# One scan for all head pairs, the range test between the masks, and a new order behind chunk 11

## The reference

```python
for t in range(S):                                   # r, k, v, w: (2, 8, 768, 48)
    cur = einsum('bhd,bhe->bhde', u[None] * kt, vt)
    y[:, :, t] = einsum('bhd,bhde->bhe', rt, state + cur)
    state = wt[:, :, :, None] * state + einsum('bhd,bhe->bhde', kt, vt)
# x: y as (2, 768, 384)
h = gelu_tanh(x @ w_in); u, v = h[..., :512], h[..., 512:]
v_s = einsum('ts,bsd->btd', w_sg, normalise(v) * g_ln) + b_sg[None, :, None]
x = x + (u * v_s) @ w_out
u2 = x + (relu(x.T @ w_tok1) @ w_tok2).T
out = u2 + relu(u2 @ w_ch1) @ w_ch2
```

## Time and profile before

| | us |
|---|---|
| median of 3 runs | 390.93 |
| lowest, highest | 390.72, 392.92 |
| the profiled execution | 391.33 |
| its span (first to last instruction) | 389.8 |
| busy: PE, DVE, POOL, ACT | 379.3, 178.7, 178.2, 105.3 |

### The profile page before, as it was taken

How to read it: one execution, slowest core, us unless ns; L and a number is a source line. 1 busy time by engine, 2 the same in 40 slices (tenths; PEclk the granted TensorE clock), 3 DMA queues, 4 the chain that set the end, 5 groups by cost and what they waited for, 6 DMA issues and landing times.

```text
span 389.8 us, 6178 instructions
## 1 busy us (share of the span) xinstructions
PE 379.3 (97%) x2380; PEld 354.8 (91%) x2380; DVE 178.7 (46%) x365; ACT 105.3 (27%) x193; POOL 178.2 (46%) x188
## 2 busy tenths in 40 slices
PE   8999699998999999999999999999999999999996
PEld 7899688897999998999999998889998899988996
DVE  6898788877644533224435753342113310133101
ACT  4457255664110204760012031340002300033000
POOL 4898889999556543966999920000000000000000
PEclk9999589998999999999999999999999999999999
DMA  8999947662102020020214300000010000100001
GB/s 237 284 290 290 251 145 215 206 214 77 66 0 83 0 83 0 2 80 2 82 41 141 102 4 0 2 0 22 20 40 2 0 21 21 40 2 0 22 20 40
DMA packets 15985, 30.69 MB, mean 79 GB/s; under 512 B 2002, under 2 KB 9555, under 8 KB 15955
## 3 DMA queue, kind: packets, MB, share of 16 engines
q1 hardware_dynamic: 15954, 30.29, 25.9%
HBM read 27.92 MB, written 2.36 MB: 78 GB/s over the span
## 4 chain that ended last, share of the span: by engine, by line
PE 96%; issue 1%; DVE 1%; POOL 1%; POOLq 0%; DVEq 0%
PE bank L1113 26%; PE bank L1114 26%; PE bank L1115 26%; PE bank L1182 5%; PE bank L1132 3%; PE bank L1178 3%; PE bank L1218 2%; PE bank L1272 2%; PE bank L1159 1%; PE bank L1140 1%; PE bank L1279 0%; DVE pre L897 0%; DVE dg L919 0%; POOL rku L568 0%; PE bank L1146 0%
## 5 line engine op out<-in xcount | busy, mean ns | idle before, releaser
L786 ACT ACTIVATE ha_hi<-bank 128x512 fp32r<-128x512 f32 x36 | 21.6, 599 | 107.7 <-PE bank L1115 107.7
L1021 DVE SCALAR_TENSOR_TENSOR ha_lo<-bank,ha_hi 128x512 fp32r<-128x512 f32 x36 | 24.9, 692 | 51.0 <-ACT ha_hi L786 51.0
L1113 PE MATMUL bank<-c_hi,ha_lo 128*128 128x384 f32 x144 | 48.2, 335 | 0.0
L1115 PE MATMUL bank<-c_hi,ha_hi 128*128 128x384 f32 x144 | 48.2, 334 | 0.0
L1114 PE MATMUL bank<-c_lo,ha_hi 128*128 128x384 f32 x144 | 48.2, 334 | 0.0
L1115 PE MATMUL bank<-u2T_hi,c_hi 128*128 128x512 f32 x108 | 42.1, 390 | 0.0
L1114 PE MATMUL bank<-u2T_lo,c_hi 128*128 128x512 f32 x108 | 42.1, 390 | 0.0
L1113 PE MATMUL bank<-u2T_hi,c_lo 128*128 128x512 f32 x108 | 42.0, 389 | 0.0
L1030 DVE TENSOR_TENSOR x<-bank,x 128x384 f32<-128x384 f32 (+1 forms) x12 | 6.5, 540 | 59.4 <-PE bank L1115 59.4
L1113 PE MATMUL bank<-sg_hi,z_lo 128*128 128x384 f32 x96 | 32.4, 337 | 0.0
L1114 PE MATMUL bank<-sg_lo,z_hi 128*128 128x384 f32 x96 | 32.1, 334 | 0.0
(11 more groups left out here) (138 smaller groups left out, 859.0 us busy)
## 6 DMA issues: line engine op xcount, KB each, us to landing
krT<-in_kr_turned SPq DMA_DIRECT2D x12, 448.0 KB, 5.8
kr<-in_kr_rows SPq DMA_DIRECT2D x12, 384.0 KB, 6.0
raw<-in_moe_w_ch SPq DMA_DIRECT2D x12, 384.0 KB, 3.2
vn<-in_v_rows SPq DMA_DIRECT2D x12, 192.0 KB, 5.5
raw<-in_moe_w_sg SPq DMA_DIRECT2D x6, 384.0 KB, 4.4
out<-x SPq DMA_DIRECT2D x11, 192.0 KB, 1.9
raw<-in_moe_w_in SPq DMA_DIRECT2D x4, 384.0 KB, 8.4
raw<-in_moe_w_tok SPq DMA_DIRECT2D x4, 384.0 KB, 3.1
```

The costliest lines, as they stand in the source:

```text
L786: sc.activation(ha[0][:, i, :], bank[:, :], ACT.Relu).then_inc(act_out, 1)
L1021: ve.scalar_tensor_tensor(ha[1][:, i, :], bank[:, :], 0.0, ha[0][:, i, :].bitcast(F32), ALU.max, ALU.subtract).then_inc(dve_out, 1)
L1113: te.matmul(dst, left[1], right[0], start=first, stop=False)
L1115: return te.matmul(dst, left[0], right[0], start=False, stop=last)
```

## The change

- **Scans.** w is stored with one more column in front of each pair (value 0), so that each pair is 129 wide (WP). `backward` is one scan over 515 elements of all four pairs, with multiply and add, where `ends` holds 1.0 at each pair's end and 0 elsewhere; `forward` is one with `starts`, whose first column per pair is 1/suf. Both lie in SBUF, and `steps` is gone. The very first backward scan is cut in two, and its w is loaded in two transfers.
- **Order in a chunk.** DVE does `forward(n + 1)` ahead of the masks; POOL's order is yt, rp, kp, rk, rku. PE's outputs are cut into the old state (`old_part`, ahead of `state_products`) and one part for each mask.
- **Range test.** In chunk 5, PE's `sum_range` follows the scores, `count_range` stands between DVE's two masks. xT products follow the outputs of chunk 5.
- **x from y.** `y_tile` writes x in every chunk, one chunk later; `x_tile`, `bound_x` and POOL's fill are gone. The other branch corrects x afterwards (`fix_x`).
- **Buffers.** Four places for krT and kr in the first chunks; a second place for the u product (uT).
- **Behind chunk 11.** The sg products of sequence 0 stand behind xT, three v and all u products of sequence 1. The splits of w_sg (2 to 5) and w_out on ACT and POOL stand after the last chunk. Normalisation and x1 splits follow the new order.

```diff
-                for p in range(NP):
-                    ve.tensor_tensor_scan(suf[0:QP, n % 2, p, 0:PART][:, ::-1], w_tile(n)[0:QP, p, :][:, ::-1],
-                                          steps[0:QP, :], 1.0, ALU.mult, ALU.bypass).then_inc(suf_done, 1)
+            def scan_back(n, first, end):
+
+                ve.tensor_tensor_scan(row(suf[:, n % 2])[:, first:end][:, ::-1], row(w_tile(n))[:, first + 1:end + 1][:, ::-1],
+                                      row(ends)[:, first:end][:, ::-1], 1.0, ALU.mult, ALU.add).then_inc(suf_done, 1)
...
-                ve.reciprocal(pre[0:QP, :, 0:1], suf[0:QP, n % 2, :, 0:1]).then_inc(inverted, 1)
+                ve.reciprocal(starts[0:QP, :, 0:1], suf[0:QP, n % 2, :, 0:1]).then_inc(inverted, 1)
...
+                ve.tensor_tensor_scan(row(pre)[:, 0:WS - 1], row(w_tile(n))[:, 0:WS - 1], row(starts)[:, 0:WS - 1], 1.0,
+                                      ALU.mult, ALU.add).then_inc(pre_done, 1)
...
-                ve.tensor_tensor(x[:, 0, n, :] if n < YR else src, src, yt[:, n % BR, :], ALU.add).then_inc(y_done, 1)
+                ve.tensor_tensor(x[:, n // NC, n % NC, :], src, yt[:, n % BR, :], ALU.add).then_inc(y_done, 1)
...
             scale_k(0)
-            scale_k(1)
             rk_products(0)
-            scale_r(1)
             rku_products(0)
-            rk_products(1)
-            for n in range(1, YR):
+            for n in range(YR):
+                if n:
+                    diagonal_v(n - 1)
+                scale_r(n + 1)
                 scale_k(n + 1)
-                rku_products(n)
-                scale_r(n + 1)
...
                 rk_products(n + 1)
-            rku_products(YR)
+                rku_products(n + 1)
...
+            forward(YR + 1)
+            mask(YR, 0)
+            count_range()
+            mask(YR, 1)
+            y_tile(YR - 1)
+            scale_k(YR + 1)
+            diagonal(YR)
+            take_slot(YR, 1)
+            backward(YR + 2)
+            take_slot(YR, 2)
...
                 else:
-                    pe.wait_ge(x_out, NCH - YR)
+                    pe.wait_ge(y_done, NCH)
...
-    (5, 0): [("xT", 0, 0), ("xT", 0, 1)], (5, 1): [("xT", 0, 2), ("v", 0, 0)], (5, 2): [("xT", 0, 3)],
+    (5, 1): [("xT", 0, 0), ("xT", 0, 1)], (5, 2): [("xT", 0, 2), ("xT", 0, 3)],
...
-TAIL = ([("sg", 0, i) for i in range(3, 8)] + [("xT", 1, i) for i in range(6)] + [("out", 0, i) for i in range(6)]
-        + [("v", 1, i) for i in range(6)] + [("u", 1, i) for i in range(8)] + [("sg", 1, i) for i in range(8)]
+TAIL = ([("xT", 1, i) for i in range(6)] + [("v", 1, i) for i in range(3)] + [("u", 1, i) for i in range(8)]
+        + [("sg", 0, i) for i in range(8)] + [("v", 1, i) for i in range(3, 6)] + [("out", 0, i) for i in range(6)]
+        + [("sg", 1, i) for i in range(8)]
```

More of the change, by code:

```diff
@@ L166, in build @@
     vn = put("vn", [PART, VR, C])
-    pre = put("pre", [PART, NP, PART])
+    pre = put("pre", [PART, NP, WP])
+    starts = put("starts", [PART, NP, WP])
+    ends = put("ends", [PART, NP, WP])
     kp = put("kp", [PART, NP, PART])
@@ L277, in w_tile, with row, krT_tile, kr_tile @@
             return wz[:, n, :, :] if n < NC else wn[:, n % WR, :, :]
+        def row(t):
+            return t[0:QP].rearrange("p a t -> p (a t)")
+        def krT_tile(n):
+            return krT_more[:, n - KR] if KR <= n < KF else krT[:, n % KR]
+        def kr_tile(n):
+            return kr_more[:, n - KR] if KR <= n < KF else kr[:, n % KR]
+        def wait_place(eng, sems, n):
+            if n < KF:
+                eng.wait_ge(sems[n], 16)
+            else:
+                eng.wait_ge(sems[n % KR], 16 * ((n - KF) // KR + 2))
+        def before(n):
+            return n - KF if n < KF + KR else n - KR
         def wait_w(eng, n):
@@ L499, in general_path, with fix_x @@
                 gp.tensor_tensor(gd[:, 1:2], gu[:, 0:1], gu[:, 0:1], ALU.add)
[L500 to L505, removed]
[L506 removed]
+            for i in range(YR):
+                fix_x(pool, gp, i)
+        def fix_x(pool, gp, i):
+            pool.wait_ge(y_done, i + 1)
+            b, c = divmod(i, NC)
+            gp.dma_start(x[:, b, c, :].rearrange("p (h d) -> p h d", h=H),
+                         y_slow[H * b:H * b + H, PART * c:PART * c + PART, :].rearrange("h p d -> p h d")
+                         ).then_inc(slow_in, 16)
+            pool.wait_ge(slow_in, 16 * EG * (B + 4 * (S // STEP)) + 16 * (i + 1))
         def pool_copy(dst, src):
@@ L628, in split_gated, with chunk @@
                                  ).then_inc(g_split, 1)
-            low = {5: [("w_in", 0)], 6: [("w_in", 1), ("w_sg", 0)], 7: [("w_sg", 1)], 8: [("w_sg", 2), ("w_sg", 3)],
-                   9: [("w_sg", 4)]}
-            first = {10: [("w_sg", 5)]}
-            def chunk(n):
-                diagonal_v(n)
-                for piece in first.get(n, []):
-                    split_low(*piece)
+            low = {6: [("w_in", 0), ("w_in", 1)], 9: [("w_sg", 0)], 10: [("w_sg", 1)]}
+            def chunk(n, slow):
+                diagonal_v(n - 1)
                 for b, i in v_jobs(n - 1):
@@ L858, in _ @@
                     take_job(kind, b, i)
-                if kind == "v" and i:
-                    normal(b, i - 1)
-                if (kind, b, i) == ("u", 1, 0):
-                    normal(1, NC - 1)
-                if (kind, b, i) == ("u", 1, 7):
-                    for tc in range(NC):
-                        x1_high(0, tc)
-                if kind == "out" and b:
-                    x1_high(1, i)
+                if kind == "xT" and i in (1, 3):
+                    split_high("w_sg", 3 + i // 2)
+                if (kind, b, i) == ("u", 1, 0):
+                    split_high("w_sg", 5)
+                if (kind, b, i) == ("u", 1, 4):
+                    split_high("w_out", 0)
+                    split_high("w_out", 1)
+                if (kind, b, i) == ("sg", 0, 7):
+                    for tc in range(3):
+                        normal(b + 1, tc)
+                if kind == "v" and i > 3:
+                    normal(b, i - 1)
+                if (kind, b, i) == ("v", 1, 5):
+                    normal(b, i)
+                if kind == "out":
+                    x1_high(b, i)
         @block.vector
@@ L1097, in _ @@
                     stats(b, i)
-                if (kind, b, i) == ("u", 1, 7):
-                    for tc in range(NC):
-                        x1_low(0, tc)
-                if kind == "out" and b and i:
-                    x1_low(1, i - 1)
-                if (kind, b, i) == ("out", 1, NC - 1):
-                    x1_low(1, i)
+                if kind == "out" and i:
+                    x1_low(b, i - 1)
+                if (kind, i) == ("out", NC - 1):
+                    x1_low(b, i)
         @block.tensor
@@ L1282, in _ @@
             spread_u()
-            keep_busy(4, ps[6])
-            for n in range(NCH):
+            keep_busy(2, ps[6])
+            for n in range(YR):
+                scores(n)
+                turn_kp(n)
+                if n:
+                    carry_state(n)
+                    old_part(n)
+                else:
+                    keep_busy(5, ps[6])
+                state_products(n)
+                new_part(n, 0)
+                new_part(n, 1)
+                keep_busy(2)
+            for n in range(YR, NCH):
                 scores(n)
```

388 lines of the change are left out of this document (190 added, 198 removed), and 12 rows, old and new, of the table SLOT.

## The result

The changed kernel takes 407.19 us (median, 405.41 to 408.61), the kernel before 391.86 us beside it: a ratio of 1.0389 with a 95% interval of 1.0333 to 1.0446. It is slower by 3.9%, where I forecast 401 us (+2.6%) and a range that ended at 406. The profiled execution took 408.61 us with a span of 407.1 and a mean granted clock of 0.962; its counterpart before has 391.33, 389.8 and 0.981. The clock that isn't granted comes to (1 - 0.962) x 407.1 = 15.5 us against 7.4 before, so up to 8 of the 17.3 us between the two spans are lost by the clock (an upper bound, since PE also stands idle in some of that time).

What follows compares the result with a forecast made beforehand. Early chunks were bound by PE, DVE, POOL and DMA together, the tail by packed matmuls. Early chunks +6.6, behind by 5.1 after the hole, y at 117.2, then tail 278.6, clock 2 and 4.0: 401.8, so 401 us; range 381 to 406.

Steps and rivals of the forecast that it cites:

- the scans are held: Long scans, with two SBUF operands, exclude POOL's products: about 1.0 us of port each; held and unabsorbed 0.53.
- not-held rival: Scans held only by POOL's own chain: chunks near 5.7 us, 383.5 us in all (-1.9%); chance 0.35.
- the price of a scan: A 515-element scan on DVE takes 1.1 us, the middle between bounds of 0.67 and 1.6.
- Chunks 0 to 4: Early chunks: scores of chunk 5 come at 44.2 us against 37.6, +6.6.
- 7.3 us a chunk: Chunks 0 to 4: POOL's products 5.1, two scans at 1.0 and 0.2 for handovers on the port.
- Hole: After chunk 5: flag at 51.3, scores of chunk 6 at about 55.5 against 52.4; behind by 5.1 in all.
- banks 6 and 7 come free only as DVE takes them: Hole after chunk 5: first xT products stand behind the outputs; scores of chunk 6 at about 55.5.
- Chunks 6 to 10: From scores of chunk 6 to those of chunk 11: 49.6 us from 58.0, scores of chunk 11 at 107.6.
- The port is wanted for 54.6 us, more than PE's 48.3: Chunks 6 to 10: POOL's 42.9 us plus DVE's nine scans 9.0 and five kp products 2.7 exceed PE's work.
- the second half absorbs it: Rival: POOL's gaps take the scans in chunks 6 to 10, only early chunks pay: 390.5 us; absorbed or mixed 0.12.
- Chunk 11 and y: After chunk 11's scores at 107.6: y at 117.2, PE stalled 3.5 us, low clock after it.
- held, and the clock falls too: Rival: 1.6 us PE idle in each of four 7.3 us early chunks also costs clock: 407 us.

Runs made afterwards that it cites:

- e1: The changed kernel with four short scans per direction again in chunks 0 to 5, second operand in PSUM: 403.61 us, ratio 1.0315.
- e11: e1 with the short scans' ones read from SBUF instead of a PSUM bank: 414.58 us, ratio 1.0550.
- e5: e4, with POOL waiting before its first two win_lo until kp of chunk 6 is done: 394.58 us, ratio 1.0034.
- e3: The changed kernel with the last piece of w_in issued in SP's round 5 instead of 6: 402.3 us, ratio 1.0284.
- e4: The changed kernel with the edits of e1 and e3 together: 396.98 us, ratio 1.0108.
- e7: e4 with yt of chunk 11 ahead of POOL's last sg_lo and z_lo: 395.23 us, ratio 1.0068.
- e2: The kernel before with only the long scans (padded w, starts and ends in SBUF): 413.77 us, ratio 1.0533.
- e8: e4 with the edits of e5 and e7, and POOL's rp and kp of chunk 1 ahead of chunk 0's rk and rku: 396.9 us, ratio 0.9996.
- e9: e8 with four filler products instead of two ahead of the first scores: 394.15 us, ratio 1.0019.

## Why the prediction was right or wrong

**Right: the scans are held.** This was the step that decided the direction. The lines above, e1 and above all e11 show it; the Trainium skill, "SBUF — State Buffer" (Who interferes with whom), counts a VectorE instruction with two SBUF inputs as a contender for GpSimd's port, and the trace agrees, now for scans too (421 ns at most, or 1335, by the place of one operand). The not-held rival needed every scan within 30 ns of one value. Without the port but with all else of the change, the time is not known, since chunks 6 to 11 kept their long scans in every experiment.

**Close: the price of a scan.** I took 1.1 us between 0.67 and 1.6; it is 1.21 to 1.23. "Some 0.5 us a chunk can be saved on DVE": the old ones cost 4 x 0.396 = 1.6 and 4 x 0.454 = 1.8 us, two new ones 2.46 when nobody holds them, so it is 0.9 us. My own 1.1 would have given 1.2; the 0.5 was the saving of one direction alone. It changed nothing in the sum, where only the held time counts.

**Chunks 0 to 4: +6.6, measured 42.78 - 37.64 = +5.1**, from other parts. "7.3 us a chunk" was a little too much: POOL's kp products are 6.9 us apart, so the two scans take 1.8 us of its time in a chunk and not 2.2. "I put chunk 1's scores at 15 us" was right for POOL, which has kp(1) ready at 15.2; PE, at the low clock in chunk 0, started on it only at 17.08. That I had not seen, but it cost nothing here, because POOL was the limit again from chunk 3 on: 15.2 + 4 x 6.9 = 42.8. The chunks themselves, which came to 6.4 us each by the scores, hide this.

**Hole: behind by 5.1, too little by 1.1.** The flag came at 47.32, not 51.3, 1.4 us of it because chunk 5 began earlier, the rest because I had added up what ran side by side: the backward scan of chunk 6 was over at 43.8, 1.0 us behind the scores, and DVE's forward scan, mask and count ran beside POOL's yt and rku products. But "banks 6 and 7 come free only as DVE takes them" was the point, and I gave kp(6), which stands ahead of them on DVE, a normal price. The hole lasts 12.4 us instead of 55.5 - 44.2 = 11.3, and scores of chunk 6 come at 55.17 where I had 55.5: two errors that cancel, which is luck. The clock behind the hole, low until 66 us, had no term in my sum at all. e5 shows that the wait for kp(6) can be taken away; what it is worth in time stays open.

**Chunks 6 to 10: the step that failed.** I had 107.6 - 55.5 = 52.1 us, and it is 116.61 - 55.17 = 61.4. Chunk 6 holds all of it and more: by an even split of my 52.1 it would take 10.4, and takes 21.5, and the four chunks behind it would take 41.7, and take 39.9. "The port is wanted for 54.6 us, more than PE's 48.3" was wrong for chunks 7 to 10: PE is busy 39.93 of 39.93 there, 10 us a chunk, and POOL's 36.1 fit in. My rival "the second half absorbs it" had this right. The step that failed is a term that I put at nothing without a reason, and that my list "Edits at nothing" doesn't even have: the table of loads. The diff moves piece 3 of the weights from entry 5 to entry 6 of `later`. I read the table as the order of work on ScalarE and POOL and gave the loads no time at all. On SP that piece is behind kr(8), and this behind a product of POOL, so the load starts 18.9 us later than before (63.86 against 44.96; in e3 it goes out by 51.3) and holds up ScalarE's queue, xT_hi, and PE. e3 against the changed kernel puts this at 7.6 us of chunk 6 and 4.9 us of the median, e4 against e1 at 2.1%, about 8 us, with intervals that lie apart: it is as large as the whole distance between 401.8 and 408.6 for the profiled execution. Another 3.7 us of chunk 6 stay without the late load (e3), at the clock of 0.59 that comes over from the hole. With the load early (e3) the ratio is 1.0284, near my 1.026; in part that is luck too, since the errors in the hole, in chunk 6's clock and in chunks 7 to 10 happen to balance.

**Chunk 11 and y: 9.6 us, measured 123.84 - 116.61 = 7.2.** The stall is there, but short: 1.01 us ahead of the last twelve transposes in the trace, where I had 3.5; e7 takes it away in its trace, and its gain lies within the noise. I had a clock behind it that adds 2, and it cost about that, 1.7: from 123.84 to the end of PE at 404.2 are 280.3 us, where I had 278.6 + 2.

**Rival "held, and the clock falls too": 407.** Its number is the measured one, its mechanism isn't. It wanted idle times of 1.6 us in each of four early chunks, and the clock is 1.00 from 20 to 45 us. The low clock lies from 8 to 14, from 53 to 66 behind the idle time in the hole, and from 70 to 76 behind the late load.

**By terms, for the profiled execution (us against the forecast of 401.8):** early chunks -1.4, hole +1.1, chunks 6 to 10 +9.3, chunk 11 -2.4, tail and what lies behind it +0.2: +6.8, and 401.8 + 6.8 = 408.6.

## What to carry to other kernels

Fewer instructions are no saving if the one that is left reads a second operand from SBUF while GpSimd works: look at where each operand of a VectorE instruction lies before counting instructions. Where VectorE has an instruction with two SBUF operands, a row of GpSimd instructions without a wait in it can hold it up for the row's whole length; a deliberate wait at that place lets it in (5.16 us became 1.56 here), and is worth a try, though its gain in time isn't shown apart. Look at the clock of each stretch too: an idle time in one place (4.6 us in the hole) was followed by a low clock in the next (0.50 for most of chunk 6). And when a diff shifts an entry in a table of loads, follow that entry through the issuing queue: find what it is queued behind and what those transfers wait for.

## What the runs showed of the hardware

- A scan over 515 elements on 112 partitions takes 1.21 to 1.23 us undisturbed, a scan of 128 takes 0.40: by the difference of the two about 2.1 ns an element and some 0.12 us fixed.
- An instruction of DVE with two SBUF operands can be held through three of POOL's in a row, two of which were issued after it: 5.16 us for 0.67, and up to 6.26 us for a scan in e2.
- With ones read from PSUM a 128-element scan varies by 32 ns, with ones read from SBUF by 942 ns, though the second operand is only bypassed in it.
- The products ahead of the first scores can run at half pace with PE never idle and the granted clock recorded as 1.00 (e8, e9, also e4 and e5: 16 score products in 2.08 us). Why, no run here tells.
